# Experts: the second layer of the previous tile as one block between a tile's first layer and the transposes of its output, and rows kept for six tiles

## What is computed

```python
def _moe_ref(x, w_skip, w_gate, w1, w2):
    out = x.copy()
    xc = x[x @ w_skip > 0]
    ...                       # e_idx: expert of each row, gate_w: its softmax weight
    for e in range(E):
        mask = e_idx == e
        h = np.maximum(xc[mask] @ w1[e], 0.0)
        y[mask] = gate_w[mask, None] * (h @ w2[e])
    out[do_compute] = xc + y
    return out
```

## Time and profile before

| | before |
|---|---|
| median of 3 runs | 502.18 us (497.6 to 502.59) |
| the profiled execution | 501.69 us |
| its span, first to last instruction | 500.0 us |
| PE busy | 463.2 us (93%) |
| granted TensorE clock, mean | 0.978 |
| expert stage, first row transpose to last `add_parts` | 109.4 to 208.0 us |
| DMA over the span | 67.27 MB, mean 135 GB/s |

### The profile page before, as it was taken

The page is one execution under the profiler, slowest core; times in us unless marked ns, Lnnn a source line. Parts: engine busy times, 40 slices in busy tenths (PEclk is TensorE's granted clock), DMA queues, the critical chain, the costliest instruction groups (busy, mean ns, idle before and its releaser), DMA issues.

```text
span 500.0 us, 10512 instructions
## 1 busy us (share of the span) xinstructions
PE 463.2 (93%) x3885; PEld 351.2 (70%) x3885; DVE 219.1 (44%) x531; ACT 194.5 (39%) x425; POOL 87.8 (18%) x136
## 2 busy tenths in 40 slices
PE   7779898678999899879999999999999999999995
PEld 6668776554544445568888888888888888888884
DVE  5567676622121221434655564443324444333332
ACT  9446654102222222414455544443324434333332
POOL 7655463022434334200000000000000000000000
PEclk9989998889999999979999999999999999999999
DMA  8989985979987079192000000210001002000002
GB/s 234 242 287 304 262 287 174 358 294 385 395 306 278 19 271 399 42 364 98 0 1 1 21 22 0 79 49 0 0 0 42 0 0 84 0 0 0 0 0 84
DMA packets 30626, 67.27 MB, mean 135 GB/s; under 512 B 3400, under 2 KB 9552, under 8 KB 30592
## 3 DMA queue, kind: packets, MB, share of 16 engines
q1 hardware_dynamic: 28960, 64.49, 38.0%
q0 software_dynamic: 1344, 1.76, 1.1%
q10 hardware_dynamic: 288, 0.52, 0.3%
HBM read 60.03 MB, written 7.73 MB: 136 GB/s over the span
## 4 chain that ended last, share of the span: by engine, by line
PE 56%; DMA 1%; DVE 0%; issue 0%; ACT 0%; DVEq 0%; POOLq 0%; SPq 0%
PE bank L1390 9%; PE bank L1391 9%; PE bank L1392 9%; PE bank L1371 9%; PE bank L1369 9%; PE bank L1370 9%; PE bank L1353 1%; PE bank L1066 1%; DMA xrow<-x_rows 1%; DMA x_rows<-y_out,sidx 0%; DVE x_sb L1025 0%; DVE stage L1036 0%; ACT x_sb L715 0%; DVEq L322 0%; POOLq L322 0%
## 5 line engine op out<-in xcount | busy, mean ns | idle before, releaser
L1390 PE MATMUL bank<-w_r,ghi 128*128 128x512 f32 x192 | 76.7, 399 | 0.0
L1391 PE MATMUL bank<-w_r,ghi 128*128 128x512 f32 x192 | 75.9, 395 | 0.0
L1392 PE MATMUL bank<-w_r,glo 128*128 128x512 f32 x192 | 75.9, 395 | 0.0
L1369 PE MATMUL bank<-x_sb,w_r 128*128 (+1 forms) x192 | 75.2, 392 | 0.7 <-DVE x_sb L1025 0.7
L1371 PE MATMUL bank<-x_sb,w_r 128*128 (+1 forms) x192 | 75.8, 395 | 0.0
L1370 PE MATMUL bank<-x_sb,w_r 128*128 (+1 forms) x192 | 75.1, 391 | 0.0
L1045 DVE TENSOR_TENSOR act_g<-act_g,clipped 128x512 f32<-128x512 f32 x48 | 33.3, 693 | 77.3 <-ACT clipped L733 77.3
L732 ACT ACTIVATE act_g<-bank,minus_c 128x512 f32<-128x512 f32 x48 | 33.0, 687 | 87.1 <-DVE clipped L1043 87.1
L1047 DVE TENSOR_TENSOR glo<-act_g,ghi 128x512 fp32r<-128x512 f32 x48 | 33.2, 692 | 34.8 <-ACT ghi L736 34.8
L1286 PE MATMUL bank<-w_f,hT 128*32 128x512 f32 x288 | 47.8, 600 | 0.1
L736 ACT ACTIVATE ghi<-act_g 128x512 fp32r<-128x512 f32 x48 | 30.3, 632 | 37.8 <-DVE act_g L1045 22.7
(11 more groups left out here) (177 smaller groups left out, 598.0 us busy)
## 6 DMA issues: line engine op xcount, KB each, us to landing
w_f<-w SPq DMA_DIRECT2D x64, 512.0 KB, 9.7
v_sb<-vW SPq DMA_DIRECT2D x8, 585.0 KB, 6.4
w_f<-w_in SPq DMA_DIRECT2D x8, 512.0 KB, 8.0
w_f<-w_out SPq DMA_DIRECT2D x8, 512.0 KB, 9.6
k_raw<-kT SPq DMA_DIRECT2D x8, 400.0 KB, 6.8
q_sb<-qT SPq DMA_DIRECT2D x16, 192.0 KB, 8.2
x_rows<-x_pair SPq DMA_DIRECT2D x8, 384.0 KB, 4.7
out<-stage SPq DMA_DIRECT2D x12, 256.0 KB, 2.3
```

The costliest lines, as they stand in the source:

```text
L1369: mm(bank[f % 2][:, :], hi, x_hi, start=(c == 0), stop=False)
L1390: mm(bank[4 + i][:, :], hi, w_hi, start=(f == 0), stop=False)
L1391: mm(bank[4 + i][:, :], hi, w_lo, start=False, stop=False)
L1392: last = mm(bank[4 + i][:, :], lo, w_hi, start=False, stop=(f == F2C - 1))
```

## The change

PE: `tile` now runs the first layer, `transpose_rows`, `add_parts`, both halves of the previous tile's `down`, and only then takes `h_set` and transposes `h_sb`, both halves into one bank. ACT copies both halves at once (`hT_set` in place of `hT_first` and `hT_second`). `add_parts` is also run once before the first tile and in the first tile. DVE: `result` stands right behind `hidden`, and `rows` and `keep_rows` behind it, for tile m + 2 in place of m + 1. So `xres` holds six tiles in place of four. POOL's and SP's code is the same. To fit, tensors are padded to 32 bytes in place of 64 and nine small routing tensors share memory with `probs`.

```diff
@@ sb @@
-        size += (-size) % 64
+        size += (-size) % 32
...
-    xres = sb("xres", [P, 4, YGRP], F32)
+    xres = sb("xres", [P, 6, YGRP], F32)
@@ ACT @@
-            def first_half():
-                take(act, htr_first)
-                s.activation(hT[:, 0, :], bank[2][:, 0:P], ACT.Copy).then_inc(hT_first, 1)
-
-            def second_half():
-                s.activation(hT[:, 1, :], bank[3][:, 0:P], ACT.Copy).then_inc(hT_second, 1)
+            def take_hidden():
+                take(act, htr_done)
+                s.activation(hT[:, :, :].rearrange("p a n -> p (a n)"), bank[2][:, 0:2 * P], ACT.Copy).then_inc(hT_set, 1)
...
-            first_half()
-            take(act, htr_second)
-            second_half()
             copy_rows()
+            take_hidden()
             with act.Fori(0, number - 1) as n:
-                first_half()
                 copy_rows()
-
                 take_parts()
-                second_half()
+
+                take_hidden()
             take_parts()
@@ DVE @@
-            dve.sem_inc(part_set, 1)
+            dve.sem_inc(part_set, 3)
...
-                v.tensor_copy(xres[:, bass.ds(n % 4, 1), :], xg[par][:, :].unsqueeze(1))
+                v.tensor_copy(xres[:, bass.ds(n % 6, 1), :], xg[par][:, :].unsqueeze(1))
...
             rows(0, 0)
             keep_rows(0, 0)
+            no_result()
+            rows(1, 0)
+            keep_rows(1, 1)
...
             hidden()
-            rows(1, 0)
-            keep_rows(1, 1)
-            hidden()
+            no_result()
             rows(0, 1)
-
-            take(dve, sum_done)
-            dve.sem_inc(y_taken, 1)
             keep_rows(2, 0)
             hidden()
+            no_result()
             rows(1, 1)
-            result(0, 0)
             keep_rows(3, 1)
             with dve.Fori(0, half - 2) as i:
+                for par in range(2):
+                    hidden()
+                    result(par, i)
+                    rows(par, i + 2)
+                    keep_rows(2 * i + 4 + par, par)
+            for par in range(2):
                 hidden()
-                rows(0, i + 2)
-                result(1, i)
-                keep_rows(2 * i + 4, 0)
-                hidden()
-                rows(1, i + 2)
-                result(0, i + 1)
-                keep_rows(2 * i + 5, 1)
-            hidden()
-
-            dve.sem_inc(xs_set, 1)
-            result(1, half - 2)
-            result(0, half - 1)
-            result(1, half - 1)
+                result(par, half - 2)
+
+                dve.sem_inc(xs_set, 1)
+            for par in range(2):
+                result(par, half - 1)
@@ PE @@
                 take(pe, xT_set)
                 up(e)
+                transpose_rows()
+                add_parts()
                 if before is not None:
-                    add_parts()
-                    take(pe, hT_first)
-                    down(before, 0)
+                    take(pe, hT_set)
+                    for half in range(2):
+                        down(before, half)
                 take(pe, h_set)
-                nc.tensor.transpose(bank[2][:, 0:P], h_sb[:, 0:P], ident[:, :]).then_inc(htr_first, 1)
-                if before is None:
-                    nc.tensor.transpose(bank[3][:, 0:P], h_sb[:, P:2 * P], ident[:, :]).then_inc(htr_second, 1)
-                else:
-                    take(pe, hT_second)
-                    nc.tensor.transpose(bank[3][:, 0:P], h_sb[:, P:2 * P], ident[:, :])
-                transpose_rows()
-                if before is not None:
-                    down(before, 1)
+                for half in range(2):
+                    last = nc.tensor.transpose(bank[2][:, half * P:(half + 1) * P], h_sb[:, half * P:(half + 1) * P], ident[:, :])
+                last.then_inc(htr_done, 1)
...
             transpose_rows()
+            add_parts()
             for e in range(EXP):
```

More of the change, by code:

```diff
@@ L147, in sparse_attention_moe_kernel @@
     tile_of = sb("tile_of", [P, BATCH * QT], F32, over)
+    nt_r = sb("nt_r", [P, EXP], F32, over)
+    nt_f = sb("nt_f", [P, EXP], F32, over)
+    cum_f = sb("cum_f", [P, EXP + 1], F32, over)
+    half_f = sb("half_f", [1, 1], F32, over)
+    half_i = sb("half_i", [1, 1], I32, over)
+    tiles_f = sb("tiles_f", [1, 1], F32, over)
+    extra_f = sb("extra_f", [1, EXP], F32, over)
+    pack_t = sb("pack_t", [1, EXP], F32, over)
+    pack_f = sb("pack_f", [1, 2], F32, over)
     probs = sb("probs", [P, 2, 4 * KEYS], F32, a)
@@ L171, in sparse_attention_moe_kernel @@
     hot_id = sb("hot_id", [P, BATCH * QT, TS], F32, a)
-    nt_r = sb("nt_r", [P, EXP], F32, a)
-    nt_f = sb("nt_f", [P, EXP], F32, a)
     cum_t = sb("cum_t", [P, EXP + 1, EXP + 1], F32, a)
-    cum_f = sb("cum_f", [P, EXP + 1], F32, a)
-    half_f = sb("half_f", [1, 1], F32, a)
-    half_i = sb("half_i", [1, 1], I32, a)
-    tiles_f = sb("tiles_f", [1, 1], F32, a)
-    extra_f = sb("extra_f", [1, EXP], F32, a)
-    pack_t = sb("pack_t", [1, EXP], F32, a)
-    pack_f = sb("pack_f", [1, 2], F32, a)
     spare = [base + 3 * 2 * UNITS * CHUNK * 4]
@@ L271, in sparse_attention_moe_kernel @@
     h_set = sem("h_set")
-    htr_first, htr_second = sem("htr_first"), sem("htr_second")
-    hT_first, hT_second = sem("hT_first"), sem("hT_second")
+    htr_done = sem("htr_done")
+    hT_set = sem("hT_set")
     sum_done = sem("sum_done")
@@ L981, in result, with no_result @@
                 v.scalar_tensor_tensor(y_out[par][:, :].unsqueeze(1), bank[6][:, 0:YGRP].unsqueeze(1), gate_all[:, bass.ds(n, 1)],
-                                       xres[:, bass.ds(n % 4, 1), :], ALU.mult, ALU.add).then_inc(y_taken, 1)
+                                       xres[:, bass.ds(n % 6, 1), :], ALU.mult, ALU.add).then_inc(y_taken, 1)
                 v.tensor_copy(sidx[par][:, :], idx_all[:, bass.ds(n, 1)]).then_inc(y_set, 1)
+            def no_result():
+                take(dve, sum_done)
+                dve.sem_inc(y_taken, 1)
             dve.wait_ge(idx_done, 1)
@@ L1335, in _ @@
             add_parts()
-            take(pe, hT_first)
-            down(EXP - 1, 0)
-            take(pe, hT_second)
-            down(EXP - 1, 1)
-            take(pe, xT_set)
+            take(pe, hT_set)
+            for half in range(2):
+                down(EXP - 1, half)
             add_parts()
```

## The result

The changed kernel takes 501.8 us (median of 20 runs, 498.2 to 506.72), the kernel before 499.42 us beside it (median of 20). The ratio is 1.0051, 95% interval 1.0026 to 1.0075: half a per cent slower, within the 1% that the prediction called no change. Forecast were 494.5 us and a range of 490 to 500; the gain of 7.2 us did not come.

What follows compares the result with a forecast made beforehand. PE, waiting for `h_sb` in the expert stage, was taken as the bound. PE's 4.46, the gather's 4.55 and the late word's 5.01 gave 4.75 us per tile for 5.23: 15 tiles save 7.2, 501.69 to 494.5 us, range 490 to 500.

Steps and rivals of the forecast that it cites:

- The wait goes, 1.0 us per tile.: PE in the expert stage: its wait for `h_set` disappears behind other work, 1.0 us per tile.
- The cover: PE's work behind the first layer, 2.3 us, against the 1.93 us that `h_sb` needs in t10.
- The gather's chain, "4.55 per tile": DVE and POOL: `y_out`, scatter, gather, its data and copies take 9.1 us for two tiles while weights load.
- L: Time from a gather's start on POOL to its data, taken as 5.3 us under weight load.
- DVE's new wait: Sign: DVE's `xs` waits on the gather's DMA in tiles under load, not between 157 and 170 us.
- The late word 5.01 in some: In some tiles `h_sb` starts no earlier than 5.01 us behind the last, PE's end being told 0.75 after the gather's.
- 4.75 as the middle: Expert-stage period forecast at 4.75 us per tile, between PE's 4.46 and the late word's 5.01.
- The rival of 498.5 us: A chain through POOL replaces the wait: every tile told late (5.01) or gathers of 6.3 (5.05); gain 3.0 us, chance 0.28.
- The start, "0, with 1 us either way": Start of the expert stage: `h_sb` of t2 comes at about 122.0 us as before, change 0, 1 us either way.
- The late word as such: While POOL issues a gather, DVE learns of PE's finished work 0.75 us after its end; layers ending before the gather escape.
- `down` in pairs of groups: Rival: `down` runs two groups at a time, each half costing 1.0 us more; 18 us slower, 520 us, chance 0.09.
- PEld's wait at the `h_sb` transpose small: Sign: PE's weight load at the first `h_sb` transpose waits little, where it waited 19.7 us before.

Runs made afterwards that it cites:

- Gather first: Changed kernel with each gather ahead of the scatter on POOL, asked for one tile earlier: 495.23 us, ratio to before 0.9913 (set 1); 493.94 us, 0.9871 (set 3).
- set 1: Runs on one chip with their own runs of the kernel before (499.4 us); there the changed kernel, unedited, took 501.99 us, ratio 1.0061.
- after, again: The changed kernel run again without an edit, against the kernel before: profile span 496.2 us, time 501.99 us, ratio 1.0061.
- set 3: Later runs on the same chip as set 1, kernel before 501.0 us; there the changed kernel, unedited, took 501.79 us, ratio 1.0007.
- the kernel with 188 instructions more: Gather first with 47 more narrow idle matmuls on PE ahead of the expert stage: 486.69 and 486.78 us, ratios to before 0.9938 and 0.9933.

## Why the prediction was wrong, point by point

The sum had 7.2 us gained between t2 and t17 and 0 at the start. The runs show 1.3 gained (5.15 per tile where 4.75 was forecast) and 2.3 or more lost at the start.

**Where the time goes.** The stage bounds the kernel, and a gain there is a gain of the whole: right. Gather first gained 8.8 us between t2 and t17 (set 1) and lost 2.5 at the start; its median fell by 4.2, in the right direction and two thirds of the 6.3, since single profiles also differ by some us ahead of the stage and behind it (the first transpose comes between 104.0 and 114.2 us).

**"The wait goes, 1.0 us per tile."** This is the first step that failed, as an account of what it is worth. The wait did go, and the time did not. The prediction had the loop in hand: it added 0.60 + 1.32 + 1.32 + 1.02 + 0.75 = 5.01 for the new order and did not hold the same sum against the old one, where the earlier trace rows gives 0.78 for its first term, 5.19 in all, and the period is 5.23. So POOL's loop, not PE, had set the pace, and the trace of before held no proof that PE would be the bound once released. The cover itself was right: 2.3 us, and with rows in time PE does 4.56 to 4.63 (forecast 4.46).

**The gather's chain, "4.55 per tile".** The second step that failed: mechanism right, sizes wrong. `y_out` follows by 0.86, not 0.60; copy to `h_sb` with the wake-up takes 1.0, not 0.55; L was taken as 5.3 with an upper bound of 6.3, and was 5.1 to 6.3 under load with 6.7 to 6.9 at the worst. 4.5 + L for two tiles, where I had 3.8 + L: 4.9 per tile at L = 5.3, 5.6 at 6.7. DVE's new wait is there as forecast, 31.8 us on the late chip, nearly all of it for gathers issued under load; in the stretch without weights PE starts a tile every 4.56 to 4.63 us. On the prompt chip this chain is what sets the long steps.

**"The late word 5.01 in some", and 4.75 as the middle.** On the late chips, where the result was measured, this was, by the count below, the larger part of the miss: 4.0 of 6.0 us. In "after, again" `h_sb` is held by the copy of rows itself in 3 of the 15 steps (to t8, t14 and t16: 5.10, 6.08 and 5.08 us). In the other 12 it starts 0.58 to 0.74 behind the gather's end, so they are rounds of POOL's loop: six of 4.76 to 4.89 us, where `y_out` follows `h_sb` by 0.5 to 0.6, and six of 5.22 to 5.44, where it follows by 0.85 to 1.09. They average 5.08, not 4.75. (In the quiet stretch PE itself keeps to 4.56, and `h_sb` falls from 0.97 to 1.74 behind its layer.) The late gathers have a hand in the long ones, as at t4: `xs` is copied at 130.53, PE transposes it at 130.99, `add_parts` behind it ends at 131.72, and `y_out` follows at 132.34, 0.85 behind `h_sb`. No run takes this apart; but with the gather first, on the same chip, the 15 steps together are 7.4 us shorter.

**The rival of 498.5 us** (chance 0.28), a chain through POOL in the place of the wait, in either form (every tile told late, or gathers of 6.3), is what happened between t2 and t17: 1.3 us gained, where it gave 3.0. Its "every tile told late (5.01)" names most of the steps, its gathers the longest ones.

**The start, "0, with 1 us either way".** The third step that failed: 2.3 us in set 1. In set 3 it was 4.2 (16.4 against before's 12.1), of which 1.3 is the lower clock in `down`. The 2.3 hold three things: PE's stall for instructions grew from 1.15 to 2.0 (the prediction took "the same stall"), t3's gather is now issued in t0, so that t0's `h_sb` is 1.2 late (0.2 before) where no `down` covers it, and the copy for t2 is late by 0.2 to 0.3. In set 1 the stage gives -1.3 + 2.3 = +1.0 us, in set 3 -1.6 + 4.2 = +2.6; medians moved by +2.6 and +0.8, and by +2.4 in the result. So stage and time agree in size, not set by set.

**The late word as such.** Right as a fact (0.6 to 0.8 behind a gather's end in most tiles, on late chips), right that there is an escape, wrong in being only the gather's and only DVE's, and it was not known that it hangs on the chip.

**`down` in pairs of groups:** did not happen; 16 records span 1.90 to 2.20 in "after, again" up to t16.

**"PEld's wait at the `h_sb` transpose small":** a poor test. It is 14.6 us even in the fastest kernel, where `h_sb` is ready 2 us ahead; about 0.8 per tile is the weight load standing behind matmuls of 512 columns. Of the 19.7 in the earlier trace rows only the rest was waiting.

What stays open: what differs between late and prompt chips, which no row names; what the kernel before looks like on a prompt chip; and how much the kernel with 188 instructions more gains on a late chip.

## What to carry to other kernels

Before a wait is removed, add up each loop that passes through the waiting point, from the rows of the kernel as it is; where one comes to the period itself, that loop may set the pace and the wait be only its slack; a run that moves the waiting engine alone tells. When a gather is asked for later, its cost is all of the steps between, the copies queued ahead of the next result too, and its latency under the heaviest load that it meets, not a middle. Compare kernels on the same chip: this change is worth +0.1 to +0.6% on one and +1.3% on another.

## What the runs showed of the hardware

- On two chips of five seen in the sets (one of them twice), what PE has finished reaches DVE and ACT only 0.6 to 0.8 us after the end of an indirect DMA that POOL is issuing, gather or scatter (each 1.02 us), in most tiles. DVE's word to PE and a DMA's word to DVE come through in the meantime. On the other three chips the same overlap costs nothing (0.19 us). The kernel before takes 10 us of 500 longer on the late chips.
- A gather of 64 KB takes 2.3 to 2.7 us from issue to data on a quiet DMA, and 5.1 to 6.9 while weights load; the worst, 6.7 to 6.9, come as a load starts anew. The Trainium skill (DMA: Bandwidth & Descriptors, "Anatomy of one DMA — SWDGE (gpsimd) path") gives a fixed 2.0 us plus the bytes' time, which only the quiet ones come near.
- PE stopped for 0.34 to 2.04 us at places that move with the length of its program, beside a 16 KB transfer on the queue of instructions; 188 instructions more moved the stop to where PE waits anyway.
- At a granted clock of 0.50 (1.2 GHz) a first layer took 3.33 us where it takes 1.93 at 1.00 (2.4 GHz). Such stretches, 3.4 us and longer, lie wholly or in part in the start of the stage in 11 of the 20 profiles, so starts are to be compared only at the same clock.
